# State sums as three products of three heads on a diagonal, and TensorE's steps taken two at a time

## The reference

```python
for t in range(S):
    m_new = np.maximum(f_gate[:, :, t] + m, i_gate[:, :, t])
    f_stab = np.exp(f_gate[:, :, t] + m - m_new)
    i_stab = np.exp(i_gate[:, :, t] - m_new)
    m = m_new
    C = f_stab * C + i_stab * einsum('bhd,bhe->bhde', v_t, k_t)
    n = f_stab * n + i_stab * k_t
    y[:, :, t] = sigmoid(o_t) * einsum('bhde,bhe->bhd', C, q_t) / maximum(abs(n . q_t), 1)
x = y as (3072, 320)
x = relu(x @ w_in)**2 @ w_out                 # layer 1
h = x @ w_in2
x = where(h > 0, h, exp(min(h, 0)) - 1) @ w_out2   # layer 2
```

## Time and profile before

| what | value |
|---|---|
| median of 3 runs | 830.93 us (830.81, 830.93, 833.44) |
| profiled execution's own time | 832.15 us |
| its span | 830.3 us, 1.85 us less than its own time |
| TensorE matmul busy | 824.3 us, 99% of the span |
| VectorE / ScalarE / GpSimd busy | 634.7 us (76%) / 492.8 us (59%) / 260.6 us (31%) |
| granted TensorE clock, whole span | 1.00 |

### The profile page before, as it was taken

How to read it: one execution, slowest core, us unless ns; L and a number is a source line. 1 busy time by engine, 2 the same in 40 slices (tenths; PEclk the granted TensorE clock), 3 DMA queues, 4 the chain that set the end, 5 groups by cost and what they waited for, 6 DMA issues and landing times.

```text
span 830.3 us, 15300 instructions
## 1 busy us (share of the span) xinstructions
PE 824.3 (99%) x5451; PEld 813.5 (98%) x5451; DVE 634.7 (76%) x1447; ACT 492.8 (59%) x1088; POOL 260.6 (31%) x270
## 2 busy tenths in 40 slices
PE   9999999999999999999999999999999999999998
PEld 7899999999999999999999999999999999999998
DVE  5798798888897988987966687777868777777642
ACT  4698675776766867678657754444444444444433
POOL 2664222322222222212102353333333333333332
DMA  7785444353653444445132300000000000000000
GB/s 250 241 229 149 136 119 110 109 132 90 160 150 80 140 119 110 109 110 147 46 105 70 106 3 4 27 4 26 2 28 3 28 3 27 4 26 5 2 24 25
DMA packets 29939, 67.64 MB, mean 81 GB/s; under 512 B 9736, under 2 KB 17064, under 8 KB 27304
## 3 DMA queue, kind: packets, MB, share of 16 engines
q1 hardware_dynamic: 29288, 65.23, 27.8%
q10 hardware_dynamic: 576, 1.44, 0.5%
HBM read 60.87 MB, written 4.03 MB: 78 GB/s over the span
## 4 chain that ended last, share of the span: by engine, by line
PE 96%; DVE 2%; DMA 1%; ACT 1%; issue 0%; POOL 0%; DVEq 0%
PE hps L1000 44%; PE acc L1014 41%; PE att L925 5%; PE att L889 2%; PE att L916 2%; PE att L905 2%; DMA wts<-m_rows 1%; ACT wts L494 1%; DVE gate L648 0%; DMA m_rows<-x 0%; DVE wts L659 0%; DMA x<-in_gates_ends 0%; PE att L930 0%; DVE x L704 0%; DVE xtl L712 0%
## 5 line engine op out<-in xcount | busy, mean ns | idle before, releaser
L1000 PE MATMUL hps<-xth,win 128*128 128x384 f32 x1280 | 351.4, 340 | 0.0
L1014 PE MATMUL acc<-wout,ghi 128*128 128x320 f32 x1536 | 345.0, 311 | 0.0
L1000 PE MATMUL hps<-xtl,win 128*128 128x384 f32 x768 | 260.2, 339 | 0.0
L1014 PEld LDWEIGHTS acc<-wout,ghi 128*128 128x128 f32 x1536 | 259.4, 188 | 0.0
L1014 PE MATMUL acc<-wout,glo 128*128 128x320 f32 x768 | 237.4, 309 | 0.0
L1000 PEld LDWEIGHTS hps<-xth,win 128*128 128x128 f32 x1280 | 230.1, 189 | 0.3
L456 POOL TENSOR_TENSOR glo<-hact,ghi 128x384 fp32r<-128x384 f32 x128 | 130.2, 1018 | 215.4 <-ACT ghi L623 215.4
L1000 PEld LDWEIGHTS hps<-xtl,win 128*128 128x128 f32 x768 | 145.0, 189 | 0.0
L1014 PEld LDWEIGHTS acc<-wout,glo 128*128 128x128 f32 x768 | 144.0, 188 | 0.0
L618 ACT ACTIVATE hact<-hact 128x384 f32<-128x384 f32 x128 | 67.4, 526 | 122.3 <-DVE hact L857 122.3
L825 DVE TENSOR_TENSOR glo<-hact,ghi 128x384 fp32r<-128x384 f32 x128 | 75.9, 593 | 66.0 <-ACT hact L580 65.1
(11 more groups left out here) (142 smaller groups left out, 729.7 us busy)
## 6 DMA issues: line engine op xcount, KB each, us to landing
raw<-in_qk SPq DMA_DIRECT2D x20, 960.0 KB, 7.1
wts<-m_rows SPq DMA_DIRECT2D x24, 512.0 KB, 8.5
kvo<-in_kvo SPq DMA_DIRECT2D x21, 484.0 KB, 7.9
x<-in_w_all SPq DMA_DIRECT2D x12, 352.0 KB, 5.5
wts<-in_w_all SPq DMA_DIRECT2D x12, 352.0 KB, 3.0
q_of_three<-in_q_trios SPq DMA_DIRECT2D x20, 180.0 KB, 2.7
out_x<-hsum SPq DMA_DIRECT2D x16, 160.0 KB, 1.9
x<-in_w_all ACTq DMA_DIRECT2D x4, 352.0 KB, 5.8
```

The costliest lines, as they stand in the source:

```text
L1000: last = nc.tensor.matmul(hps[t % 2][:, 0:NT], win[:, j, w, :], x[:, kk, :], start=(i == 0), stop=(i == len(parts) - 1))
L1014: last = nc.tensor.matmul(acc[u][:, 0:DM], g[t % GR][:, cols], wout[:, j, w, :], start=(j == 0 and i == 0), stop=(j == NF - 1 and i == 2))
```

## The change

It has two parts.

**State sums.** `state_added` takes three heads at once: the stationary side is 120 columns of k (80 for the last two heads), the moving side 123 columns (82), so 3 fp32 products, 6 instructions. Only the diagonal blocks of the result are wanted. The states live on that diagonal for good, as [120, 3, 123] tiles; `first_state` and `update_state` take one operation for each position on the diagonal, three instead of one, with a mask column `of_head` that is 1 on the block's rows and 0 elsewhere. The three state DMAs and `state_diag` go. The decay moves from VectorE to GpSimd (`decay_state`, 120 x 369, at start + 3), and `update_state` moves from ahead of `add_inter` to behind `finish`. The decay factors are spread once over 120 partitions by three DMAs. `from_state` reads 123 and 82 columns where it read 126 and 84.

**Pairs.** From block 1 on TensorE takes steps in twos: both first products, the attention work of both steps, then two second products. Between the first products of a block's last pair and those of the next block's first pair stand three second products (the two of the last pair and one ahead of the new pair); in the pair of steps 2 and 3 there is only one. `empty_acc` moves one step forward, in layer 2 behind L623.

```diff
-        state = [sb(f"state_{i}", [D, H, EV]) for i in range(B)]
+        state = [sb(f"state_{i}", [ROWS, TRIOS, 3 * E]) for i in range(B)]
-        state_diag = sb("state_diag", [ROWS, TRIOS, 3 * EV])
+        of_head = sb("of_head", [ROWS, 3])
+        new_states = A2[0:ROWS, 0:TRIOS * 3 * E].rearrange("d (i n) -> d i n", i=TRIOS)
+        def heads_in_trios(t, i):
+            return t[:, 0:len(range(i, H, 3)), i * E:(i + 1) * E]
...
# SyncE
-            def load_state(g):
-                wait(sp, "state_ready", g - B + 1)
+            def load_trios(g):
                 wait(sp, "inter_ps", with_state(g))
...
-                for i in range(3):
-                    n = len(range(i, H, 3))
-                    dst = state_diag[i * D:(i + 1) * D, 0:n, i * EV:(i + 1) * EV]
-                    sp.dma_start(dst, src[:, i:H:3, :]).then_inc(s["state_in"], 16)
                 sp.dma_start(q_of_three[:], q_trios[g]).then_inc(s["trio_in"], 16)
...
# GpSimd, at start + 3
+            def decay_state(g):
+                pool.wait_ge(s["decay_in"], 48)
+                pool.wait_ge(s["inter_ps"], with_state(g) + 1)
+                st = state[batch_of(g)]
+                part = decay[:, chunk_of(g) - 1, batch_of(g), :].unsqueeze(2).broadcast_to([ROWS, TRIOS, 3 * E])
+                nc.gpsimd.tensor_tensor(st[:], st[:], part, ALU.mult).then_inc(s["decayed"], 1)
...
# VectorE
             def update_state(g):
...
-                nc.vector.tensor_tensor(st, st, part, ALU.mult).then_inc(s["decayed"], 1)
                 dve.wait_ge(s["decayed"], with_state(g) + 1)
                 dve.wait_ge(s["dc_ps"], g + 1)
-                nc.vector.tensor_tensor(st, st, new, ALU.add).then_inc(s["state_ready"], 1)
+                for i in range(3):
+                    st = heads_in_trios(state[batch_of(g)][:], i)
+                    done = nc.vector.scalar_tensor_tensor(out=st, in0=heads_in_trios(new_states, i), scalar=of_head[:, i:i + 1], in1=st,
+                                                          op0=ALU.mult, op1=ALU.add)
+                done.then_inc(s["state_ready"], 1)
...
                         if g is not None:
-                            update_state(g)
                             add_inter(g)
...
                             finish(g)
+                            update_state(g)
...
# ScalarE, layer 1 and layer 2
-                        if j == LAG - 1 and block > 0:
+                        if j == LAG - 2 and block > 0:
                             empty_acc(block - 1)
...
-                        if j == LAG - 1:
-                            empty_acc(block - 1)
                         act.wait_ge(s["g_ready"], t + 1)
                         act.wait_ge(s["g_used"], T * (t - GR + 1))
                         nc.scalar.activation(ghi[t % GR][:], gfull[t % 2], ACT.Copy).then_inc(s["ghi_ready"], 1)
+                        if j == LAG - 2:
+                            empty_acc(block - 1)
...
# TensorE
-                for h in range(H):
-                    last = nc.tensor.matmul(A2[0:D, h * E:(h + 1) * E], k_of(g)[:, h, :], wv[:, h, :], start=True, stop=True)
+                for i in range(TRIOS):
+                    n = min(3, H - 3 * i)
+                    last = nc.tensor.matmul(new_states[0:n * D, i, 0:n * E], k_of(g)[:, 3 * i * D:(3 * i + n) * D],
+                                            wv[:].rearrange("t h e -> t (h e)")[:, 3 * i * E:(3 * i + n) * E], start=True, stop=True)
...
+            for block in range(1, 2 * BLOCKS):
+                for j in range(0, NF, 2):
                     t = NF * block + j
-                    if j == 0 and block > 0:
+                    if j == 0:
                         second_product(t - LAG)
                     first_product(t)
...
+                    first_product(t + 1)
+                    attention(t)
+                    attention(t + 1)
+                    if j != 2:
+                        second_product(t - LAG + (j == 0))
+                    second_product(t - LAG + 1 + (j == 0))
```

More of the change, by code:

```diff
@@ L19 @@
 E = D + 1
-EV = D + 2
 NF = FF // P
@@ L120, in mlstm_two_dense_layers @@
         int_col = sb("int_col", [P, CH, R])
-        decay = sb("decay", [D, CH, R])
+        decay_sent = sb("decay_sent", [D, 3, CH - 2, B, TRIOS])
+        decay = sb("decay", [ROWS, CH - 2, B, TRIOS])
         last = sb("last", [P, B, H])
@@ L317, in _ @@
             load_m(4)
+            spread_decay()
             for n in range(RING + 3, FROM_ACT):
@@ L449, in _ @@
                             split_q_lo(g, 1)
+                        g = tile_at(t, 3)
+                        if g is not None and 0 < chunk_of(g) < CH - 1:
+                            decay_state(g)
                         if t + EARLY < NF:
@@ L664, in update_state @@
                     return
-                st = state[batch_of(g)][:, :, 0:E]
-                new = A2[0:D, 0:H * E].rearrange("d (h e) -> d h e", e=E)
-                dve.wait_ge(s["decay_ready"], 1)
-                wait(dve, "state_in", 48 * (with_state(g) + 1))
-                part = decay[:, chunk_of(g), heads_of(g)].unsqueeze(2).broadcast_to([D, H, E])
-                nc.vector.tensor_tensor(st, st, part, ALU.mult).then_inc(s["decayed"], 1)
+                dve.wait_ge(s["consts"], 5 + B)
                 dve.wait_ge(s["decayed"], with_state(g) + 1)
                 dve.wait_ge(s["dc_ps"], g + 1)
-                nc.vector.tensor_tensor(st, st, new, ALU.add).then_inc(s["state_ready"], 1)
+                for i in range(3):
+                    st = heads_in_trios(state[batch_of(g)][:], i)
+                    done = nc.vector.scalar_tensor_tensor(out=st, in0=heads_in_trios(new_states, i), scalar=of_head[:, i:i + 1], in1=st,
+                                                          op0=ALU.mult, op1=ALU.add)
+                done.then_inc(s["state_ready"], 1)
             def add_inter(g):
@@ L803, in _ @@
             nc.vector.tensor_copy(int_col[:, CH - 1, :], acc[2][:, P + R:P + 2 * R]).then_inc(s["int_ready"], 1)
-            nc.vector.tensor_copy(decay[:, 1:CH - 1, :].rearrange("d c r -> d (c r)"), acc[2][0:D, 2 * P:3 * P]).then_inc(s["decay_ready"], 1)
+            dve.wait_ge(s["consts"], 6 + B)
+            for i in range(3):
+                src = acc[2][0:D, 2 * P:3 * P].rearrange("d (c b h) -> d c b h", b=B, h=H)[:, :, :, i:H:3]
+                done = nc.vector.tensor_copy(decay_sent[:, i, :, :, 0:len(range(i, H, 3))], src)
+            done.then_inc(s["decay_ready"], 1)
             for n in range(POOL_LO, EARLY):
@@ L915, in from_state @@
                     n = min(3, H - 3 * i)
-                    last = nc.tensor.matmul(A0[:, 3 * i * EV:(3 * i + n) * EV], q_of_three[0:n * D, i, :],
-                                            state_diag[0:n * D, i, 0:n * EV], start=True, stop=True)
+                    last = nc.tensor.matmul(A0[:, 3 * i * E:(3 * i + n) * E], q_of_three[0:n * D, i, :],
+                                            state[batch_of(g)][0:n * D, i, 0:n * E], start=True, stop=True)
                 last.then_inc(s["inter_ps"], 1)
@@ L1019, in second_product, with attention @@
                     last.then_inc(s["g_used"], T)
-            for block in range(2 * BLOCKS):
-                for j in range(NF):
+            def attention(t):
+                block, j = divmod(t, NF)
+                if t in FIRST_STATES:
+                    state_added(FIRST_STATES[t])
+                g = tile_at(t, 0)
+                if g is not None:
+                    scores(g)
+                g = tile_at(t, 2)
+                if g is not None:
+                    if g > T:
+                        state_added(g)
+                    from_state(g)
+                g = tile_at(t, 3)
+                if g is not None:
+                    within(g)
+                if block == BLOCKS - 1 and j in X2_STEPS:
+                    w = X2_STEPS.index(j)
+                    x2_transposed(w, w)
@@ L1023, in _ @@
+            for t in range(NF):
+                first_product(t)
+                attention(t)
+                if t >= LAG:
+                    second_product(t - LAG)
+                g = transposed_at(t)
+                if g is not None:
+                    x1_transposed(g)
+            for block in range(1, 2 * BLOCKS):
+                for j in range(0, NF, 2):
                     t = NF * block + j
-                    if j == 0 and block > 0:
+                    if j == 0:
                         second_product(t - LAG)
@@ L1040, in _ @@
-                    if block == BLOCKS - 1 and j in X2_STEPS:
-                        w = X2_STEPS.index(j)
-                        x2_transposed(w, w)
-                    if t >= LAG and j > 0:
-                        second_product(t - LAG)
-                    g = transposed_at(t)
-                    if g is not None and g < 2 * T:
-                        x1_transposed(g)
+                    first_product(t + 1)
+                    attention(t)
```

(3 more changed lines are left out.)

61 lines of the change are left out of this document (28 added, 33 removed).

## The result

The changed kernel is **slower**: 840.4 us, median of four runs (839.38 to 841.25), against 831.7 (830.81 to 833.44) for the kernel before on the same chip; 1.0104 times as long, 95% interval 1.0087 to 1.012. The forecast was 827.7, a gain, with a range up to 833.0: the time moved the other way, and lies above the range.

What follows compares the result with a forecast made beforehand. TensorE bounds the kernel, 85% of its chain the two dense products. Savings of 6.4 and 2.1 make 8.5 us, less waits of 3.8 and 1.5: 3.2 off 832.15, 828.95, as a median 827.7; range 822.4 to 833.0.

Steps and rivals of the forecast that it cites:

- State sums: Attention tiles on TensorE: new sums save 0.35 us a tile on 16 tiles, 6.4 us together with block 0 and from_state.
- The lower end: State sums: the 0.26 us gap comes with any change from dense products to this sum, leaving 0.16 a tile, 2.9 in all.
- rival (c): State sums: the gap around the sum stays with the new form, total 831.2 us; chance 0.14.
- the estimate by which the group itself would gain nothing: State sums, by the Trainium skill's weight-load rule: 0.53 us for the old loads and 0.53 for the new.
- Pairs on TensorE: Dense products from block 1 on: pairing saves 0.14 us a block, 2.1 us over fifteen blocks.
- What pairs cost in layer 2: TensorE waits for VectorE's maximum: 0.47 us in each of blocks 8 to 14, 0.5 on top in block 8, together 3.8.
- The price of `x2_lo`: Layer 2, VectorE: a step with this split takes 3.69 us, giving TensorE a wait of 0.30 ahead of first product 13.
- The 0.1 us for the first tile's step 7 in layer 1: A wait of about 0.1 us ahead of the first product of step 7, 5 times, 0.5 us in all.
- What they cost in layer 1: Pairs, VectorE's turns behind finish and the update: 4 waits of 0.25 us at block starts plus 0.5 elsewhere, together 1.5.
- Rival (d): VectorE's queue: the three update operations take 1.65 us together, turns come 0.95 later at 9 places, 836.3 us; chance 0.14.
- I am wrong altogether if TensorE waits for GpSimd: The prediction's own sign of complete failure, which also named TensorE waiting for ScalarE's L623 or a DMA.
- What costs nothing: Decay on GpSimd, spread_decay, first_state, empty_acc and dropped DMAs: no cost counted; the decay was to run in idle time.

Runs made afterwards that it cites:

- pairs_l1: The changed kernel with steps one at a time in layer 2, so pairs in layer 1 only, empty_acc back there too: 837.47 us, 1.0071 of before.
- sums_only: The changed kernel's new state sums without pairs, TensorE's order and empty_acc as before the change: 827.88 us, 0.9955 of before.
- q_thin: The changed kernel, but GpSimd's two products for q's low part cover 8 of 128 tokens of each head: 828.38 us, 0.9962 of before.
- pairs_only: The kernel before with TensorE's steps in pairs and empty_acc moved, old state path kept: 842.57 us, 1.0133 of before.
- sums_dve: New state sums without pairs, with the decay back on VectorE just ahead of update_state's sums instead of on GpSimd: 825.84 us, 0.9935 of before.
- pairs_l2: The changed kernel with steps one at a time in layer 1, so pairs in layer 2 only, empty_acc back there too: 831.1 us, 0.9995 of before.
- upd_first: The changed kernel with update_state ahead of add_inter again instead of behind finish: 839.62 us, 1.0083 of before.
- copy_psum: The changed kernel with finish's last copy replaced by two narrow products that read PSUM, ahead of the product of 320: 843.66 us, 1.0132 of before.
- third8: The changed kernel with the third tile of a block started at step 8, not 9: 844.17 us, 1.0146 of before.
- sums_dve_copy: New state sums without pairs, decay on VectorE, finish's last copy replaced by two products that read PSUM: 832.14 us, 1.0 of before.

## Why the prediction was wrong

**State sums: right.** L933 has 120 instructions, no wait on "issue", and stands in the chain with 0.57 against the old 0.74; a tile saves 0.34 of TensorE's time. The lower end (2.9 us in all) and rival (c) are refuted, and so is the estimate by which the group itself would gain nothing. The chain of the changed kernel:

```profile
192.13 0.57 PE att L933 x6
192.70 0.82 PE att L945 x6
193.52 2.67 PE acc L1044 x18
```

**Pairs on TensorE: right.** Block 7 has no wait and takes 44.41 instead of 44.54: 0.13, where 0.14 was forecast.

**What pairs cost in layer 2: right in size, and in place but for block 8.** 0.4 more a block, where 0.33 was forecast, and 0.9 in block 8 as against 0.83; 3.3 us measured net for blocks 8 to 14, 2.8 forecast. What block 8 has on top was expected at steps 0 to 3, from ScalarE's splits; no wait stands there, and 0.4 of the 0.5 stand ahead of step 9. Why there, no run tells. The price of `x2_lo` held because its row was read with GpSimd beside it, as it runs in both kernels: VectorE's 1.06 started at 579.60, GpSimd's product at 579.23. The 0.1 us for the first tile's step 7 in layer 1 didn't show: no gap between matmuls stands there.

**What they cost in layer 1: this is the step that failed.** The forecast had 1.5 us of waits there, 0.5 net of what the pairs save; pairs_l1 against sums_only measured 9.6. The prediction took `finish` at 2.19 and L644 at 1.22 from a stretch in which GpSimd did nothing until 260.06, and kept these durations while it moved the work. Measured in the changed kernel: from the start of `finish` (200.72) to the turns (206.53) 5.81, where 2.19 + 0.7 + 1.22 + 0.48 = 4.6 was forecast. The update was near its estimate (0.80 for 0.7). The rest is GpSimd. Instead of 4 waits of 0.25 there are 5 of 1.2 (1.352 from matmul to matmul, where 0.15 is usual), 4 more of 0.33 ahead of the third tile's scores (0.507 where 0.17 is usual), where L851 took 1.68 at 181.96 behind GpSimd's 181.93, and small ones beside them. The fifth wait stands ahead of block 6, whose third tile has no update at all. A block of layer 1 came to 57.35, where the terms of the forecast make 55.7: with block 5, some 8 of the 11.6 us between forecast and measured span. Block 0 holds another 3.0.

Why does GpSimd come just then? In a pair both first products are done ahead of the attention group. ScalarE splits q behind its work on the second of them, so it no longer waits for a first product behind `within`. ScalarE's timeline, before and after; TensorE goes on behind `within` at 198.04 and 200.51:

```profile
201.05 0.49 ACT L576 ACTIVATE hact<-hps 128x384 f32<-128x384 f32 x1 [2.11 <-PE hps L1000]
...
202.41 1.04 ACT L473 ACTIVATE q<-raw 120x1024 fp32r<-120x1024 f32 x1
```
```profile
199.93 0.47 ACT L599 ACTIVATE hact<-hps 128x384 f32<-128x384 f32 x1
...
201.28 1.04 ACT L494 ACTIVATE q<-raw 120x1024 fp32r<-120x1024 f32 x1
```

The split comes 3.9 behind the start of `finish` before (202.41 - 198.50) and 0.6 after (201.28 - 200.72). The q products follow it, and land on the copy and k's low part. This is read from the timelines: q_thin shows that GpSimd's products make the loss, but no run moved them to another time. One rule of the Trainium skill fits what the rows show: "SBUF — State Buffer", Who interferes with whom, says that a VectorE instruction with two inputs in SBUF, or a copy in a two-port mode, shares a port pair with a GpSimd instruction that reads SBUF, and that the one that issues first holds it to its end. The trace agrees: the update with one input in PSUM took 0.80 with GpSimd and without, and a start 0.01 behind GpSimd cost 1.14, one 0.29 ahead of it nothing. It agrees less with a hold to the very end: by that k's low part, 1.22 alone, would end 1.22 behind GpSimd, and it ended 1.08 to 1.09 behind. The rows show the durations and not the port.

The trace before had shown it. Groups by line, the kernel before: a copy that takes 0.20 alone has a mean three times that.

```profile
L707 DVE COPY x<-x 128x64 f32<-128x64 f32 x24 | 14.7, 613 | 0.8
```

One by one it is plainer still. In block 3 the copies of the first and second tile ran beside GpSimd's q products (219.66 to 222.19 and 237.60 to 240.13), and only the third tile's, the one that the prediction priced, ran alone:

```profile
221.64 0.61 DVE L707 COPY x<-x 128x64 f32<-128x64 f32 x1
239.05 1.14 DVE L707 COPY x<-x 128x64 f32<-128x64 f32 x1
```

Rival (d) was slower, by VectorE's queue, but by the update's price, which was 0.80 where it needed 1.05; its mechanism was wrong, though its sign came true: the turned tokens' wait is near 1 us. "I am wrong altogether if TensorE waits for GpSimd": in layer 1 it does, at one remove, and the releaser named in the rows is VectorE all the same. The one long wait whose row names GpSimd, 1.4 for `wv` in block 0, is there with the old sums as well (0.9 in pairs_only), so it doesn't decide the case.

**What costs nothing: wrong for the decay.** It was priced by its own idle engine. In block 0 GpSimd also splits `wout` and VectorE `win`; with the decay there, k's low part took 1.82 instead of 1.22 and the scores of tile 5 came 1.57 late instead of 0.28. Block 0 lost 2.4, where 0.6 was to be gained. Moving the decay back gave 2.0 in the traces, of which 0.4 is shown to be its own. The rest is TensorE's clock: over the six microseconds that begin in that wait sums_only was granted 0.72 on average, some of them at 1.2 GHz, and sums_dve 1.00, 2.4 GHz throughout, behind a wait of 1.20. In the changed kernel 9 matmuls behind the wait stand 0.27 apart instead of 0.15, which is 1.1 us. The wait alone doesn't bring the slow stretch: pairs_l2 went on at 1.00 behind the same 1.57. What decides stays open, and so does the rest of block 0's loss: the wait of 1.20 is still there with the decay back on VectorE.

In blocks 1 to 4 the decay holds VectorE up too: k's low part of the first and second tile took 1.71 beside it instead of 1.22. In sums_only TensorE waits for nothing there all the same; with pairs, this half microsecond lies ahead of the L851 that met GpSimd at 181.96, and no run has pairs with the decay on VectorE. `first_state`, the DMAs and `spread_decay` show in no wait of TensorE that the kernels with the old sums don't have too.

## What to carry to other kernels

A duration holds only beside the neighbours it was read with. If a change shifts one engine's work against another's, lay the timelines of VectorE and GpSimd over each other in their new order, and price each operation that meets the other at its worst row (here a copy of 0.20 with a mean of 0.61), not at its best. Where a saving ahead of a meeting point doesn't arrive, read the end of the work it met: here the turns began 1.59 behind GpSimd's end in four kernels, whatever came before. And time the halves of a change by themselves: one was worth 3.7 us, and 5.5 with the decay back on VectorE (part of that a matter of the clock), and the other took 12.5.

## What the runs showed of the hardware

The blocked operation ends later than the blocker by less than its full length: k's low part, 1.22 alone, ended 1.08 to 1.09 behind GpSimd in five kernels (the changed one, pairs_only, upd_first, copy_psum, third8), whenever it had started. GpSimd pays as well, but little: its two products took 2.54 alone, 2.67 and 2.85 beside VectorE's (sums_dve, sums_dve_copy). The same wait of TensorE (1.57) was followed by a stretch at 1.2 GHz in sums_only and by none in pairs_l2, and of five waits of 2.0 in third8 one was. I had expected neither that a start 0.01 apart would be worth a full 1.1 us, nor that an edit which takes a copy from VectorE, and gives it two narrow products for it, would make the kernel slower by 3.3 (copy_psum) and 6.3 (sums_dve_copy).
